# Nineteen tiny products whose results nobody reads, put into TensorE's instruction stream at two places, four warm-up products taken out

## What is computed

```python
def _attn_ref(q, k, v, alpha):              # 4 x 8 heads, 768 steps, head dimension 48
    for t in range(S):
        state = alpha[:, :, t, :, None] * state + np.einsum('bhd,bhe->bhde', k[:, :, t], v[:, :, t])
        y[:, :, t] = np.einsum('bhd,bhde->bhe', q[:, :, t], state)

def _moe_ref(x, w_in, w_out):               # 3072 tokens, 384 -> 2048 -> 384
    h = x @ w_in
    sp = np.where(h > 20.0, h, np.log1p(np.exp(np.minimum(h, 20.0))))
    return (h * np.tanh(sp)) @ w_out

def _moe2_ref(x, w_in, w_out):
    h = x @ w_in
    return (h * np.cos(h)) @ w_out
```

## Time and profile before

| | us |
|---|---|
| median of 3 runs | 865.24 |
| lowest, highest | 864.85, 866.35 |
| the profiled execution's own time | 865.5 |
| its span (first to last instruction) | 863.6 |
| TensorE busy | 854.9 (99%) |
| TensorE's share of the chain that ended last | 97% |

### The profile page before, as it was taken

The page is one execution under the profiler, slowest core; times in us unless marked ns, Lnnn a source line. Parts: engine busy times, 40 slices in busy tenths (PEclk is TensorE's granted clock), DMA queues, the critical chain, the costliest instruction groups (busy, mean ns, idle before and its releaser), DMA issues.

```text
span 863.6 us, 15910 instructions
## 1 busy us (share of the span) xinstructions
PE 854.9 (99%) x6288; PEld 706.5 (82%) x6288; DVE 428.8 (50%) x702; ACT 415.5 (48%) x732; POOL 340.4 (39%) x272
## 2 busy tenths in 40 slices
PE   8999999999999999999999999999999999999998
PEld 7778888888888888888888888888888888888886
DVE  8886342333324323300033766666666665665664
ACT  3644333333333333333456665565565555655654
POOL 5556343544344544423464433333333333333332
PEclk9999999999999999999999999999999999999999
DMA  8755553344444334310431200200200200200001
GB/s 298 237 151 173 135 175 101 92 132 115 127 113 143 92 96 137 105 29 21 135 92 55 74 1 1 74 1 1 74 1 0 74 1 0 74 1 1 37 1 38
DMA packets 72042, 69.25 MB, mean 80 GB/s; under 512 B 38432, under 2 KB 54048, under 8 KB 71968
## 3 DMA queue, kind: packets, MB, share of 16 engines
q1 hardware_dynamic: 71824, 68.10, 26.4%
q10 hardware_dynamic: 144, 0.13, 0.0%
HBM read 46.71 MB, written 13.63 MB: 70 GB/s over the span
## 4 chain that ended last, share of the span: by engine, by line
PE 97%; DVE 1%; issue 1%; ACT 0%; POOL 0%; DVEq 0%; ACTq 0%; POOLq 0%
PE low L622 45%; PE low L593 35%; PE pair L593 11%; PE pair L563 1%; PE pair L547 1%; PE low L498 1%; PE low L470 1%; PE low L430 1%; DVE growth L868 0%; PE top L470 0%; PE top L498 0%; DVE suffix L854 0%; DVE probs L912 0%; PE pair L451 0%; PE pair L517 0%
## 5 line engine op out<-in xcount | busy, mean ns | idle before, releaser
L1083 POOL TENSOR_TENSOR g_lo<-g,g_hi 128x512 fp32r<-128x512 f32 x191 | 250.8, 1314 | 480.1 <-ACT g_hi L737 479.4
L593 PE MATMUL low<-x_parts,w_hi 128*128 128x512 f32 x864 | 245.0, 392 | 0.6 <-issue 0.6
L622 PE MATMUL low<-g_hi,w_hi 128*128 128x512 f32 x576 | 224.6, 390 | 0.3 <-DVE x_out L971 0.3
L622 PE MATMUL low<-g_hi,w_lo 128*128 128x512 f32 x576 | 224.2, 389 | 0.0
L593 PEld LDWEIGHTS low<-x_parts,w_hi 128*128 128x128 f32 x864 | 160.6, 188 | 34.6 <-issue 0.5
L737 ACT ACTIVATE g_hi<-g 128x512 fp32r<-128x512 f32 x192 | 120.7, 628 | 116.4 <-PE low L622 115.6
L622 PE MATMUL low<-g_lo,w_hi 128*128 128x512 f32 x576 | 165.8, 389 | 0.0
L622 PEld LDWEIGHTS low<-g_hi,w_hi 128*128 128x128 f32 x576 | 108.1, 188 | 23.9 <-DVE x_out L971 0.7
L622 PEld LDWEIGHTS low<-g_lo,w_hi 128*128 128x128 f32 x576 | 108.0, 188 | 22.6
L622 PEld LDWEIGHTS low<-g_hi,w_lo 128*128 128x128 f32 x576 | 108.1, 188 | 22.4
L593 PE MATMUL low<-x_parts,w_lo 128*128 128x512 f32 x432 | 121.5, 390 | 0.0
(11 more groups left out here) (112 smaller groups left out, 793.5 us busy)
## 6 DMA issues: line engine op xcount, KB each, us to landing
w_raw<-w_in SPq DMA_DIRECT2D x32, 384.0 KB, 3.2
shared<-aqk_in SPq DMA_DIRECT2D x21, 512.0 KB, 4.2
v_sb<-v_in SPq DMA_DIRECT2D x24, 256.0 KB, 5.0
shared<-aqk_in SPq DMA_DIRECT2D x23, 258.0 KB, 3.6
mid<-x_out SPq DMA_DIRECT2D x6, 768.0 KB, 4.0
shared<-mid SPq DMA_DIRECT2D x6, 768.0 KB, 6.0
turned<-probs SPq DMA_DIRECT2D x64, 64.0 KB, 2.2
kd_t<-turned SPq DMA_DIRECT2D x16, 256.0 KB
```

Source lines behind the costliest of these rows:

```text
L593: mm = nc.tensor.matmul(bank, wp[:, f, k * P:(k + 1) * P], xp[:, j % 2, k, :], start=(n == 0), stop=(n == 3 * KT - 1))
L622: mm = nc.tensor.matmul(acc[m], wp[:, f, DM + m * P:DM + (m + 1) * P], gp[:, tile % GB, :], start=(f == 0 and n == 0), stop=(f == FT - 1 a ...
L1083: nc.gpsimd.tensor_tensor(g_lo[:, tile % GB, :], g[:, tile % GB, :], g_hi[:, tile % GB, :].bitcast(F32), ALU.subtract).then_inc(glo_ready, 1)
```

## The change

A new helper `spare(n, bank)` issues n products with 32 rows of contraction, 32 columns of weights and one column of data, all from the constant `ones`, into column 480 of a bank; what they write there is never read. The products have no wait and raise no semaphore.

- Ahead of chunk 1's scores, 2 warm-up products stand in place of 6, followed by 15 tiny ones.
- In chunk 16's visit, 4 tiny ones stand between `halves_update` and `inner`.

```diff
+            def spare(n, bank):
+
+                for _ in range(n):
+                    nc.tensor.matmul(bank[0:32, 480:481], ones[0:32, 0:32], ones[0:32, 0:1], start=True, stop=True)
+
...
                     halves_update(c)
+                    if c == 16:
+                        spare(4, banks[1])
                     if next_turned(c) is None:
                         inner(c)
...
             turn(1)
-            warm(6)
+            warm(2)
+            spare(15, banks[2])
             scores(1)
```

## The result

| | before | changed |
|---|---|---|
| median of 20 runs each | 865.47 us | 864.50 us |
| lowest, highest | 864.75, 866.72 | 863.48, 865.45 |
| ratio (95% interval) | | 0.9987 (0.9981 to 0.9993) |
| span of the profiled execution | 863.6 | 861.9 |

The gain is 0.97 us where 1.34 was forecast, clear of the noise of twenty runs and under the 0.2% that the chances were given for. In a second comparison (11 runs of the changed kernel) it was 0.9985 (0.9976 to 0.9994). The forecast time was 863.9 us; 864.50 lies inside both ranges given. Of the 0.60 us between, 0.37 is gain that did not come, and 0.23 is the median of before, 865.24 in three runs and 865.47 in twenty.

What follows compares the result with a forecast made beforehand. TensorE, busy 99% of the span, was taken as the bound; -1.62 us for three page-end gaps, +0.28 for chunk 16's tiny products and 0 for the opening stage gave -1.34, so 863.9 us, range 863.0 to 865.5.

Steps and rivals of the forecast that it cites:

- the 0.2% that the chances were given for: Whole kernel: 0.2% (1.73 us) tells from no change; faster below 863.5 us 0.24, slower above 867.0 0.06, the rest 0.70.
- both ranges given: Whole kernel's time: the forecast's own range 863.1 to 864.7 us, and 863.0 to 865.5 to be held 8 times in 10.
- chunk 5's visit at -50: Chunk 5's visit: page beginning moved from -6 to 50 numbers ahead of its start, claimed to remove a 0.33 us gap.

Runs made afterwards that it cites:

- the kernel with all visits at page ends: Kernel before plus some 1,280 hidden waits, so a page begins 9 numbers ahead of each visit of chunks 7 to 19; 878.14 us, ratio 1.0146.

## What to carry to other kernels

Where an engine at its limit shows idle time released by "issue", count its instructions between two such places; if the counts are multiples of one number, it is the code that is late. One such gap here was not (chunk 5's in the kernel with all visits at page ends), and only its number told. A page is a fixed number of instructions, so the danger is where many short instructions follow each other and a page begins at their start; what must be moved is that place, and instructions hidden behind long work (here satisfied waits) moved it at no cost that could be seen, while real work put among short products is paid for. After any such shift, look at every other page end, the opening stage's too, and don't credit a gap that was seen once.

## What the runs showed of the hardware

In the 24 gaps of over 0.3 us at page ends in all profiles (21 in visits of chunks 7 to 19, two in chunk 5's, the one at number 450) TensorE's restart can be held against the last packet of its instruction queue. The packet is on its way for 0.92 to 1.90 us, and TensorE goes on 1.20 to 1.58 us after its end, every time. In the kernel with all visits at page ends, the shortest gap (0.89, chunk 17) and the second longest (1.42, chunk 13) had packets of 0.96 and 1.54 us. The packet for chunk 13 started at 201.55, 0.23 us into the visit, and none of that queue (q8) starts in the second part of the gap, 203.10 to 204.45, where the view lists one queue alone:

```profile
DMA  1011000101011000000000000000004999507379
...
q1 hardware_dynamic: 88, 0.06, 26.6%
```

In the 21 gaps of chunks 7 to 19, from the start of a page's first pass to the use of the next page 2.4 to 4.5 us pass: 0.1 to 1.5 until the packet starts, 0.9 to 1.9 for it, 1.2 to 1.6 behind it. A visit uses a page in 1.9 us. The start of the packet is not tied to the page's beginning alone: it came 3.8 to 4.4 us behind it in chunk 5's visit at -50, and among long products of before up to 4.9 us ahead of it. What sets it, and what fills the last part, is open.

Also not expected: the moment at which the opening warm-up reaches its faster pace differs between executions enough to move the whole kernel by up to 1 us (first mask 9.6 to 10.6 us), which is as much as the change brings. A single profile of each kernel would have said 1.7 us.
